# One level of Strassen in the first channel product of a fused attention and mixer kernel, with its weights streamed through a ring

## The chip, the cores and the metric

The kernel runs on one core of one Trainium2 chip. The metric is the device time of one execution in microseconds (us). The kernel before has a median of 504.48 us over 3 runs (504.46 to 504.53). Five engines work in a core: TensorE (PE, matrix products into the banks of PSUM), VectorE (DVE), ScalarE (ACT), GpSimd (POOL) and SyncE (SP, which here issues the DMAs). Each engine takes its own instructions in their written order and waits on counting semaphores.

## The reference, cut to what matters

```
attn_out = local-and-global attention(q, k, v)                # 2 batches, 8 heads, 768 tokens, 64 wide
x  = attn_out as (2, 768, 512)
h  = relu(x^T @ w_tok1) @ w_tok2                              # 768 -> 256 -> 768, over tokens
u  = x + h^T
x2 = u + relu(u @ w_ch1) @ w_ch2                              # 512 -> 1536 -> 512, over channels
theta = x2 @ w_theta
y  = w_tok_r @ (x2*cos(theta)) + w_tok_i @ (x2*sin(theta))    # over tokens
u2 = x2 + y
out = u2 + relu(u2 @ w_ch)
```

The change is in the two channel products of the third step, `u @ w_ch1` (the first) and `relu(...) @ w_ch2` (the second).

## The kernel before, in words

Every product of two fp32 matrices in these stages is made of three matmuls of fp32r operands (`three`, line 285): each operand is split into a high part (rounded by a copy) and a low part (the operand minus the high part), and high*high, high*low and low*high are added up in PSUM. Splitting is work of the other engines: POOL splits the weights (a copy at line 650, a subtraction at 651), ACT makes the high part of an activation and DVE the low part.

Work runs in this order, batch 0 then batch 1 inside each stage where not said otherwise. **Attention** (both batches, `head_scores`, `transpose_probs`, `weigh_values`). **Tokens**: `hidden_tokens` (6 tiles of 128 tokens times 2 halves j) and `mixed_tokens` (8 tiles (c, k_) of 128 channels by 384 tokens, two products each); after each tile DVE adds x in the bank (line 1114), ACT rounds it (799) and DVE makes its low part (1108). **Channels**: per batch 24 steps, one for each half c of the tokens (SC = 384 columns) and each tile f of the 1536 hidden channels. `hidden(i)` is 12 matmuls of 384 columns into bank 6 or 7; ACT applies relu and rounds (806), DVE makes the low part (1123), into a ring of three; `reduce_hidden(i - 1)` is 12 matmuls of 384 columns that add into banks 0 to 3. At the end of a half, `take_h2` (1041, out of PSUM, adding the high part of u) and `finish_x2` (1047, adding the low part) give x2. The tail of a batch's tiles (`tile_to_hi`, `tile_to_lo`) for the next stage is made inside this loop, and so is the work on the first angle (`angles(0)`, `find_angles(0)`, `multiply_x(0)`) in batch 1. **Angles and mixing**: for each of 12 tiles g, `angles(g + 1)` (12 matmuls of 512 columns) and then `mix(g)` (two halves of 24 matmuls, half of them 512 and half 256 columns wide). Beside it DVE runs `find_angles(g)` (six instructions, lines 1056 to 1066), waits for two sines of ACT (771, 772), multiplies by x (1076, two instructions), ACT rounds both products (784), DVE makes their low parts (1081) and then the low part of the tile after the next (`tile_to_lo`, 1032). `mix(0)` waits until all of `take_h2` is done. **Last channels**: `last_channels`, with POOL and DVE sharing the low parts.

The weights lie in SBUF in ten slots `wsplit` of 2 x 1536 columns; they come through two staging buffers `wraw`. SP loads chunk i when chunk i - 2 has been split (`load_weight`, 487). All of w_ch1 (4 slots) and w_ch2 (4 slots) is split once, in batch 0, and stays for batch 1. The six chunks of w_tok_r and w_tok_i are rounded by ACT (`round_tokri`, 767) in slots that come free during the last half of batch 1, with POOL's subtraction (651) behind each; the two chunks of w_ch are split by POOL in the mixing stage.

Two of the lines that the text refers to by what they read:

```
dve.tensor_tensor(tile_at(g)[:, 1]..., rows_at(act_raw[:, b], s), tile_at(g)[:, 0]..., ALU.subtract)        # 1032: both operands in SBUF
dve.tensor_tensor(lo_[:, u_cols(i)], U_BANK[i][:, 0:SC], hi[:, u_cols(i)].bitcast(F32), ALU.subtract)       # 1108: one in PSUM, one in SBUF
```

## Time and profile before

| | |
|---|---|
| median of 3 runs | 504.48 us |
| the profiled execution, its own time | 504.67 us |
| its span | 502.9 us |
| TensorE busy | 496.2 us, 99% of the span, 2977 matmuls |
| VectorE busy | 271.5 us, 54% |
| ScalarE busy | 175.5 us, 35% |
| GpSimd busy | 141.5 us, 28% |
| granted TensorE clock | 1.00 of full speed |

The span is the time from the first to the last recorded instruction; about 1.8 us of the execution lie around it. Busy times are summed per engine. The mean duration of a matmul is longer than its share of the engine's time, because matmuls are pipelined: the pace is read from the starts of groups in the timeline.

### The profile page before, as it was taken

Reading aid. Unit: us, or ns where it says so; the run is one execution under the profiler, and the core shown is the slowest. Engines: PE = TensorE matmul, PEld = TensorE weight load, DVE = VectorE, ACT = ScalarE, POOL = GpSimd, SP = SyncE. Lnnn points to the kernel's source line nnn. Section 1 sums busy time; section 2 is a strip of 40 time slices with the busy share of each in tenths; the row PEclk is TensorE's granted clock in tenths of the full one; section 3 lists DMA queues with packets and bytes.
Section 4 is the critical chain, followed back from the end, with each engine's and each line's share of the span. In section 5 each row is a group of like instructions: output and inputs, shape, how many; then the busy total and the mean of one; then the engine's idle time right before and its main releaser. Section 6 shows DMA issues by size and latency. Waiting matters only on the chain.

```text
span 502.9 us, 8110 instructions
## 1 busy us (share of the span) xinstructions
PE 496.2 (99%) x2977; PEld 467.9 (93%) x2977; DVE 271.5 (54%) x715; ACT 175.5 (35%) x375; POOL 141.5 (28%) x131
## 2 busy tenths in 40 slices
PE   7999999999999999999999999999999999999997
PEld 5999999899999999989999999998888899888897
DVE  6998998672212421075212424247787665764452
ACT  6999898541111111123111143422323320321130
POOL 3575566499900000005000041730320220000040
PEclk9999999999999999999999999999999999999999
DMA  6887774634431100002120212320001221000002
GB/s 236 321 297 246 236 216 133 204 127 134 159 98 27 45 2 0 1 0 81 45 60 4 61 30 99 125 84 1 1 2 48 61 82 64 1 0 1 1 33 94
DMA packets 24777, 43.50 MB, mean 86 GB/s; under 512 B 3104, under 2 KB 17440, under 8 KB 24736
## 3 DMA queue, kind: packets, MB, share of 16 engines
q1 hardware_dynamic: 24736, 42.96, 26.8%
q8 instruction: 24, 0.39, 0.3%
q14 instruction: 17, 0.14, 0.1%
HBM read 33.52 MB, written 3.15 MB: 73 GB/s over the span
## 4 chain that ended last, share of the span: by engine, by line
PE 97%; DVE 1%; DMA 1%; issue 0%; ACT 0%
PE bank L288 74%; PE bank L1456 7%; PE bank L1236 5%; PE bank L1266 4%; PE bank L1269 4%; PE bank L1250 2%; PE bank L1248 2%; DMA counts<-both_counts 1%; PE bank L1276 0%; DVE wsplit L875 0%; DVE wsplit L946 0%; DVE act_raw L1209 0%; ACT probsT L673 0%; ACT wsplit L680 0%; DVE scores L866 0%
## 5 line engine op out<-in xcount | busy, mean ns | idle before, releaser
L288 PE MATMUL bank<-hid,wsplit 128*128 128x384 f32 x576 | 109.2, 339 | 0.0
L288 PE MATMUL bank<-split,wsplit 128*128 128x384 f32 x576 | 109.0, 339 | 0.0
L288 PE MATMUL bank<-wsplit,zs 128*128 128x512 f32 (+1 forms) x576 | 103.3, 338 | 0.0
L288 PEld LDWEIGHTS bank<-wsplit,zs 128*128 128x128 f32 x576 | 89.8, 188 | 14.2
L288 PEld LDWEIGHTS bank<-hid,wsplit 128*128 128x128 f32 x576 | 101.9, 188 | 0.3 <-DVE hid L1123 0.2
L288 PEld LDWEIGHTS bank<-split,wsplit 128*128 128x128 f32 x576 | 102.1, 188 | 0.1
L1123 DVE SCALAR_TENSOR_TENSOR hid<-bank,hid 128x384 fp32r<-128x384 f32 x48 | 26.8, 558 | 135.7 <-ACT hid L806 135.7
L651 POOL TENSOR_TENSOR wsplit<-wraw,wsplit 128x1536 fp32r<-128x1536 f32 (+1 forms) x19 | 62.8, 3308 | 76.2 <-ACT wsplit L767 75.1
L806 ACT ACTIVATE hid<-bank 128x384 fp32r<-128x384 f32 x48 | 23.5, 490 | 146.7 <-PE bank L288 146.6
L650 POOL CAST wsplit<-wraw 128x1536 fp32r<-128x1536 f32 (+1 forms) x13 | 17.4, 1338 | 125.9 <-PE bank L288 117.3
L582 POOL TENSOR_TENSOR wsplit<-qk_raw,wsplit 64x256 fp32r<-64x256 f32 x46 | 38.0, 826 | 34.0 <-DVE wsplit L883 33.6
L660 POOL TENSOR_TENSOR split<-act_raw,split 128x384 fp32r<-128x384 f32 x12 | 12.5, 1073 | 109.5 <-ACT split L840 109.5
L724 ACT ACTIVATE probs<-scores,nmax 128x232 f32<-128x232 f32 (+1 forms) x96 | 39.9, 465 | 2.4 <-DVE nmax L987 2.2
L771 ACT ACTIVATE zb<-zb 128x512 f32<-128x512 f32 x12 | 7.6, 632 | 87.4 <-DVE zb L1066 87.4
L288 PE MATMUL bank<-wsplit,tile 128*128 128x512 f32 x144 | 35.6, 395 | 0.0
L987 DVE CUSTOM_DVE_ANT_0 scores<-bank,bias 128x232 f32<-128x232 f32 (+1 forms) x96 | 32.4, 374 | 4.9 <-PE bank L1236 4.0
L1236 PE MATMUL bank<-wsplit 128*128 128x232 f32 (+1 forms) x192 | 32.7, 292 | 2.1 <-DVE wsplit L875 1.3
L1456 PE MATMUL bank<-split,wsplit 128*128 128x384 f32 x192 | 33.9, 337 | 0.0
L1266 PE MATMUL bank<-vt,probsT 128*128 128x65 f32 x192 | 33.8, 264 | 0.1
L1456 PEld LDWEIGHTS bank<-split,wsplit 128*128 128x128 f32 x192 | 33.5, 188 | 0.2
L288 PEld LDWEIGHTS bank<-wsplit,tile 128*128 128x128 f32 x144 | 26.4, 188 | 5.5
L1269 PE MATMUL bank<-vt,probsT 104*128 104x65 f32 x160 | 30.9, 275 | 0.0
(104 smaller groups left out, 599.8 us busy)
## 6 DMA issues: line engine op xcount, KB each, us to landing
wraw<-weights SPq DMA_DIRECT2D x16, 768.0 KB, 4.1
qk_raw<-qk SPq DMA_DIRECT2D x23, 528.0 KB, 4.3
vt<-v SPq DMA_DIRECT2D x10, 520.0 KB, 4.7
xT<-turned SPq DMA_DIRECT2D x64, 48.0 KB, 2.0
out<-act_raw SPq DMA_DIRECT2D x16, 192.0 KB, 1.9
wraw<-weights SPq DMA_DIRECT2D x4, 512.0 KB, 3.4
xT<-turned_early SPq DMA_DIRECT2D x16, 96.0 KB, 2.3
xT<-wraw SPq DMA_DIRECT2D x32, 48.0 KB, 1.9
```

The costliest lines, as they stand in the source:

```text
L288: mm = pe.matmul(dst, lhs(a), rhs(c), start=first and i == 0, stop=last and i == 2, skip_group_check=True)
L582: pool.tensor_tensor(q_split[D:P, n % 2, heads], q_in[D:P, n % 2, heads], q_split[D:P, n % 2, heads].bitcast(F32), ALU.subtract).then_inc( ...
L650: link(pool.tensor_copy(w_at(slot, 0, 0, width), raw))
L651: pool.tensor_tensor(w_at(slot, 1, 0, width), raw, w_at(slot, 0, 0, width).bitcast(F32), ALU.subtract).then_inc(w_ready, 1)
L724: act.activation(probs[:, n % 2, h, first:], scores[:, m % 2, e, first:], ACT.Exp, bias=nmax[:, n % 2, h:h + 1], scale=-1.0).then_inc(exp_ ...
L806: act.activation(r1s[:, i % 3, 0], bank[6 + i % 2][:, 0:SC], ACT.Relu).then_inc(r1_hi, 1)
L987: dve.tensor_tensor_reduce(out=scores[:, m % 2, e, first:], in0=S_BANK[m % 2][e][:, first:WIN], in1=bias[:, h, first:], scale=-SCALE, scal ...
L1123: dve.scalar_tensor_tensor(r1s[:, i % 3, 1], bank[6 + i % 2][:, 0:SC], 0.0, r1s[:, i % 3, 0].bitcast(F32), ALU.max, ALU.subtract).then_inc ...
L1236: mm = pe.matmul(S_BANK[m % 2][e][:, first:WIN], q_split[:, n % 2, h, :], k_split[:, i, h, key:key + WIN - first], start=i == 0, stop=i == 1)
L1266: mm = pe.matmul(dst, probsT[:, m % 2, at + P:at + 2 * P], vt[:, n % 2, 0, cols], start=m % 2 == 0 and e == 0, stop=n % T == 0, skip_group ...
L1269: mm = pe.matmul(dst, probsT[0:SEEN, m % 2, at:at + P], vt[0:SEEN, n % 2, 1, cols], start=False, stop=True, skip_group_check=True)
L1456: return pe.matmul(bank[at][:, 0:SC], w_at(CHAN_AT[k_ // 2], w, k_ % 2 * DM + d * P, P), S_(u, k_, c * SC, SC), start=first, stop=last, sk ...
```

## The change

Notation: a pair i is the two hidden tiles i and i + 6 (PAIR_F = 6 pairs). The first product of a pair over all 768 tokens is a 2 x 2 block product: the pair's two tiles by the two halves of the 512 input channels, times the two halves of the input channels by the two halves c of the tokens.

- Pair 0 of each batch is computed as before, in four products of 12 matmuls (`REGULAR`). Pairs 1 to 5 use Winograd's form of Strassen's algorithm: seven products of 6 matmuls of 384 columns instead of 48 matmuls, in banks 6 and 7.
- The four sums T1 to T4 of the blocks of u (8 tiles of 128 x 384) are made once a batch: DVE finds each (`find_sum`), ACT rounds it (`sum_to_hi`), DVE makes its low part (`sum_to_lo`). ACT copies six of the tiles of u out of PSUM for that (`u_raw`).
- The four sums of the weights are made for each pair by POOL in `split_first` (4 additions of 256 columns, copies of 768 and 1024 columns, subtractions of 768 and 1024).
- The results are put together by DVE (four additions a pair) before relu: p1 is copied out by ACT; u2, u3 and c22 are written to SBUF, the other two to PSUM. ACT's relu and DVE's low part follow, four of each a pair as before. The low part of c22 reads two operands in SBUF.
- The second product goes over all 768 tokens in blocks of six matmuls, three of 512 and three of 256 columns, into banks 0 to 5; one block of pair i - 1 stands behind each of the seven products of pair i. `take_h2` and `finish_x2` are 8 each a batch (512 and 256 columns) in place of 8 of 384.
- The weights of a pair (1024 columns of w_ch1, 1024 of w_ch2) are streamed through rings of two places, once for each batch, so they are loaded and split twice. The chunks of w_theta come between pairs 1 and 2 of batch 1.
- `angles(0)` stands behind the last of the products of batch 1, ahead of the last eight blocks. `find_angles(0)`, `sines(0)` and `multiply_x(0)` move behind it. The first two `round_tokri` are done there too, the other four one by one in the mixing stage, between `z_to_hi(g, 1)` and `tile_to_hi`.

```diff
+            def split_first(n, raw):
+                if n % PAIR_F == 0:
+                    link(pool.tensor_copy(mixes(n, 0, 0, 4), raw))
+                    return pool.tensor_tensor(mixes(n, 1, 0, 4), raw, mixes(n, 0, 0, 4).bitcast(F32), ALU.subtract)
+                a11, a12, a22, a21 = (raw[:, q * 2 * P:(q + 1) * 2 * P] for q in range(4))
+                s1, s2, s3, s4 = (mix_raw[:, q] for q in range(4))
+                link(pool.tensor_tensor(s1, a21, a22, ALU.add))
+                pool.tensor_tensor(s3, a11, a21, ALU.subtract)
+                link(pool.tensor_tensor(s2, s1, a11, ALU.subtract))
+                pool.tensor_copy(mixes(n, 0, 0, 3), raw[:, 0:3 * 2 * P])
+                link(pool.tensor_tensor(s4, a12, s2, ALU.subtract))
+                sums = mix_raw[:, :].rearrange("p q c -> p (q c)")
+                link(pool.tensor_copy(mixes(n, 0, 3, MIXES), sums))
+                pool.tensor_tensor(mixes(n, 1, 0, 3), raw[:, 0:3 * 2 * P], mixes(n, 0, 0, 3).bitcast(F32),
+                                   ALU.subtract)
+                return pool.tensor_tensor(mixes(n, 1, 3, MIXES), sums, mixes(n, 0, 3, MIXES).bitcast(F32),
+                                          ALU.subtract)
...
-                if slot < CH2:
-                    act.wait_ge(r1_ready, CHS - NF + 3 * (slot - CH1 + 1))
-                else:
-                    act.wait_ge(h2_done, CHS - NF + 3 * (slot - CH2 + 1))
+                act.wait_ge(r1_ready, B * PRODUCTS)
+                act.wait_ge(h2_done, B * BLOCKS - 2 * KD)
...
                     act.activation(split[:, 0, u_cols(i)], U_BANK[i][:, 0:SC], ACT.Copy).then_inc(uT_hi, 1)
+                    if i < 6:
+                        act.activation(u_raw[:, i], U_BANK[i][:, 0:SC], ACT.Copy).then_inc(u_copied, 1)
+                    if i == 5:
+                        sum_to_hi(0)
+                        sum_to_hi(1)
...
+            round_tokri(0)
+            round_tokri(1)
+            sines(0)
+            z_to_hi(0, 0)
...
                     z_to_hi(g, 1)
+                    if g + 2 < len(TOKRI_AT):
+                        round_tokri(g + 2)
                     if g + 2 < B * T:
                         tile_to_hi(B * T + g + 2)
...
                 for i in range(OUTB):
                     dve.wait_ge(h_ready, b * OUTB + i + 1)
                     dve.tensor_tensor(by_quads(U_BANK[i][:, 0:SC]), by_quads(U_BANK[i][:, 0:SC]), xT_at(i),
                                       ALU.add).then_inc(u_done, 1)
-                    if i:
+                    if i and i != 6:
                         lo_of_u(i - 1)
+                    if i == 5:
+                        lo_of_u(5)
+                        find_sum(0)
+                        find_sum(1)
+                    if i == 6:
+                        sum_to_lo(0)
                 lo_of_u(OUTB - 1)
+                sum_to_lo(1)
+
+                for i, (f, c) in enumerate(REGULAR):
+                    if i < 3:
+                        find_sum(2 * i + 2)
+                        find_sum(2 * i + 3)
+                    dve.wait_ge(r1_hi, b * PARTS + i + 1)
+                    dve.scalar_tensor_tensor(r1_at(b * PAIR_F, f, 1, c * SC, SC), bank[6 + i % 2][:, 0:SC], 0.0,
+                                             r1_at(b * PAIR_F, f, 0, c * SC, SC).bitcast(F32), ALU.max,
+                                             ALU.subtract).then_inc(r1_lo, 1)
+                    if i < 3:
+                        sum_to_lo(2 * i + 2)
+                        sum_to_lo(2 * i + 3)
...
+            find_angles(0)
+            take_h2(B - 1, 0)
+            take_h2(B - 1, 1)
+            multiply_x(0)
+            z_to_lo(0, 0)
+            for i in range(2, 2 * KD):
+                take_h2(B - 1, i)
             z_to_lo(0, 1)
             tile_to_lo(B * T + 2)
-            for d in range(KD):
-                finish_x2(B - 1, NC - 1, d)
+            for i in range(2 * KD):
+                finish_x2(B - 1, i)
...
+                for i, (f, c) in enumerate(REGULAR):
                     if f == 0:
                         pe.wait_ge(uT_lo, b * OUTB + (c + 1) * KD)
+                    if i >= 2:
+                        pe.wait_ge(r1_lo, b * PARTS + i - 1)
...
+                for i in range(1, PAIR_F):
+                    wait_weight(pair_in_order(b, i, 0))
+                    pe.wait_ge(r1_lo, parts - 1)
+                    product(i, 0, 6, quarter(0, 0), False)
+                    block(i - 1, *blocks[0])
+                    pe.wait_ge(p1_copied, m + 1)
+                    product(i, 1, 6, quarter(2, 0), True)
+                    block(i - 1, *blocks[1])
+                    pe.wait_ge(r1_lo, parts)
+                    pe.wait_ge(t_lo, b * SUMS + 6)
+                    product(i, 4, 7, summed(2), False)
+                    block(i - 1, *blocks[2])
...
+                if b == B - 1:
+                    angles(0)
+                for d in range(KD):
+                    block(PAIR_F - 1, 1, d)
```

## Rows read from the trace of the kernel before

**Rows 1.** The page: busy time by engine, granted clock by slice, the chain that ended last.

```profile
PE 496.2 (99%) x2977; PEld 467.9 (93%) x2977; DVE 271.5 (54%) x715; ACT 175.5 (35%) x375; POOL 141.5 (28%) x131
...
PEclk9999999999999999999999999999999999999999
...
PE 97%; DVE 1%; DMA 1%; issue 0%; ACT 0%
```

**Rows 2.** Groups of PE instructions, shapes apart: the two channel products.

```profile
L288 PE MATMUL bank<-hid,wsplit 128*128 128x384 f32 x576 | 109.2, 339 | 0.0
L288 PE MATMUL bank<-split,wsplit 128*128 128x384 f32 x576 | 109.0, 339 | 0.0
```

**Rows 3.** Timeline of PE: start us, us, then the merged instructions.

```profile
1.45 5.22 PE L1276 MATMUL bank<-wsplit 128*128 128x512 f32 x13 [1.45 <-DVE wsplit L853]
...
110.57 4.40 PE L288 MATMUL bank<-split,wsplit 128*128 128x384 f32 x24
...
142.37 2.28 PE L288 MATMUL bank<-split,wsplit 128*128 128x384 f32 x12
144.49 2.28 PE L288 MATMUL bank<-hid,wsplit 128*128 128x384 f32 x12
...
345.06 2.97 PE L288 MATMUL bank<-wsplit,tile 128*128 128x512 f32 x12
347.87 8.64 PE L288 MATMUL bank<-wsplit,zs 128*128 128x512 f32 x48
356.34 2.97 PE L288 MATMUL bank<-wsplit,tile 128*128 128x512 f32 x12
```

**Rows 4.** Timeline of DVE behind the mixing of batch 0.

```profile
106.14 0.56 DVE L1108 TENSOR_TENSOR split<-bank,split 128x384 fp32r<-128x384 f32 x1
106.61 0.56 DVE L1114 TENSOR_TENSOR bank<-bank,xT 128x384 f32<-128x384 f32 x1
...
111.72 1.21 DVE L1108 TENSOR_TENSOR split<-bank,split 128x384 fp32r<-128x384 f32 x2
```

**Rows 5.** Groups of ACT instructions, shapes apart.

```profile
L799 ACT ACTIVATE split<-bank 128x384 fp32r<-128x384 f32 x16 | 7.8, 492 | 11.7 <-DVE bank L1114 11.7
L767 ACT ACTIVATE wsplit<-wraw 128x1536 fp32r<-128x1536 f32 x6 | 8.9, 1479 | 2.9 <-DMA wraw<-weights 2.9
```

**Rows 6.** Groups of POOL instructions, shapes apart.

```profile
L651 POOL TENSOR_TENSOR wsplit<-wraw,wsplit 128x1536 fp32r<-128x1536 f32 x15 | 52.5, 3505 | 75.8 <-ACT wsplit L767 75.1
L651 POOL TENSOR_TENSOR wsplit<-wraw,wsplit 128x1024 fp32r<-128x1024 f32 x4 | 10.3, 2570 | 0.3
L650 POOL CAST wsplit<-wraw 128x1024 fp32r<-128x1024 f32 x4 | 4.2, 1042 | 117.3 <-PE bank L288 117.3
L611 POOL TENSOR_TENSOR wsplit<-wraw,wsplit 128x256 fp32r<-128x256 f32 x5 | 3.6, 727 | 0.4
```

**Rows 7.** Timelines of DVE and POOL where the two met: batch 1's channel stage.

```profile
298.67 1.31 DVE L1032 TENSOR_TENSOR tile<-act_raw,tile 128x512 fp32r<-128x512 f32 x1
...
295.92 3.52 POOL L651 TENSOR_TENSOR wsplit<-wraw,wsplit 128x1536 fp32r<-128x1536 f32 x1 [59.03 <-ACT wsplit L767]
```

**Rows 8.** Timelines of DVE and POOL where the two met: mixing stage.

```profile
353.91 2.90 DVE L1076 TENSOR_TENSOR zb<-xT,zb 128x512 f32<-128x512 f32 x1
...
353.52 2.73 POOL L651 TENSOR_TENSOR wsplit<-wraw,wsplit 128x1024 fp32r<-128x1024 f32 x1
```

**Rows 9.** Timeline of DVE, POOL idle or beside it: one step of the mixing stage, first to last.

```profile
337.05 1.96 DVE L1047 TENSOR_TENSOR act_raw<-act_raw,split 128x384 f32<-128x384 f32 x4
338.93 0.68 DVE L1056 TENSOR_SCALAR za<-bank 128x512 f32<-128x512 f32 x1
...
342.28 0.43 DVE L1066 TENSOR_SCALAR zb<-zb 128x512 f32<-128x512 f32 x1
344.02 0.69 DVE L1076 TENSOR_TENSOR zc<-xT,zc 128x512 f32<-128x512 f32 x1 [1.31 <-ACT zc L772]
...
346.62 0.69 DVE L1032 TENSOR_TENSOR tile<-act_raw,tile 128x512 fp32r<-128x512 f32 x1
```

More of the change, by code:

```diff
@@ L78, with pair_chunks, pair_in_order @@
 BORROWED = 5
-ORDER = [0, 1, 2, 6, 3, 7, 4, 8, 5, 9] + list(range(10, 20))
+def pair_chunks(first, last):
+    return [n for i in range(first, last) for n in (2 + 2 * i, 3 + 2 * i)]
+ORDER = ([TOK1, TOK2] + pair_chunks(0, PAIR_F) + pair_chunks(0, 2) + [THETA, THETA + 1]
+         + pair_chunks(2, PAIR_F) + list(range(TOKRI, CHAN + 2)))
+THETA_IN = ORDER.index(THETA)
+TOKRI_IN, CHAN_IN = ORDER.index(TOKRI), ORDER.index(CHAN)
+def pair_in_order(b, i, second):
+    return 2 + 2 * PAIR_F * b + 2 * i + second + (2 if b and i >= 2 else 0)
 BESIDE = [1, 3]
@@ L1050, in find_angles @@
             def find_angles(g):
-                theta = bank[6 if g else 4][:, :]
+                theta = bank[6][:, :]
                 dve.wait_ge(th_ready, g + 1)
@@ L1394, in _, with block @@
-                hidden(0)
-                for i in range(1, CHB):
-                    hidden(i)
-                    reduce_hidden(i - 1)
-                    if b == B - 1 and i == EARLY:
-                        angles(0)
+                def block(i, f, d):
+                    n = b * PAIR_F + i
+                    first, last = i == 0 and f == 0, i == PAIR_F - 1 and f == 0
+                    if d == 0:
+                        wait_weight(pair_in_order(b, i, 1))
+                        pe.wait_ge(r1_lo, b * PARTS + 2 * NC * i + (3 + f if i == 0 else 4 - f))
+                    if first:
+                        pe.wait_ge(t_lo, b * SUMS + 5 + d)
+                    three(pe, bank[d][:, :], lambda a: second_at(n, a, f * DM + d * P, P),
+                          lambda a: r1_at(n, f, a, 0, 512), first, last)
+                    mm = three(pe, bank[4 + d // 2][:, d % 2 * 256:(d % 2 + 1) * 256],
+                               lambda a: second_at(n, a, f * DM + d * P, P),
+                               lambda a: r1_at(n, f, a, 512, S - 512), first and d % 2 == 0, last)
+                    mm.then_inc(h2_done, 1)
@@ new lines, in product, with quarter, summed @@
+                def product(i, mix, at, rhs, more):
+                    for kk in range(2):
+                        mm = three(pe, bank[at][:, 0:SC], lambda a: mix_at(b * PAIR_F + i, a, mix, kk),
+                                   lambda a: rhs(a, kk), kk == 0 and not more, kk == 1)
+                    mm.then_inc(r1_ready, 1)
+                def quarter(k_, c):
+                    return lambda a, kk: S_(a, k_ + kk, c * SC, SC)
+                def summed(t):
+                    return lambda a, kk: sum_at(t, kk, a)
@@ L1403, in _ @@
                     hidden_tokens(b + 1, 0, 1).then_inc(tile_used, 1)
[L1404 removed]
+                for d in range(KD):
+                    block(PAIR_F - 1, 0, d)
             def mix(g):
```

424 lines of the change are left out of this document (280 added, 144 removed).

## The prediction, made blind

> **What bounds the kernel now.** I read the page's busy times and its chain first, then the groups of PE by shape, and last the timelines of the engines at the places that the change touches. TensorE is busy for 99% of the span and is 97% of the chain that ended last [rows 1]: the kernel is one unbroken stream of matmuls. So a removed matmul is worth its whole pace, and any new wait of TensorE is paid in full. Everything else is hidden at present: VectorE 54%, GpSimd 28%. The question is whether it stays hidden where the change puts its new work.
>
> **Removed: matmuls.** Each batch has 5 pairs with 7 x 6 = 42 matmuls in place of 48, so 5 x 6 x 2 = 60 of the 576 of the first product go [rows 2]. Twelve matmuls of 384 columns start 2.12 us apart (142.37 to 144.49), 0.1767 us each [rows 3]: 60 x 0.1767 = **-10.6 us**. The second product keeps its 576 matmuls, half now 512 and half 256 wide; 48 matmuls of just that mix took 8.47 us (347.87 to 356.34), 0.1765 each [rows 3]. So no change there: 0, and if the alternation costs or saves 1%, 2 us either way over the whole channel stage.
>
> **Streaming the weights.** Per pair GpSimd has four additions of 256 columns (4 x 0.73), copies of 768 and 1024 (about 0.8, between the 1024 copy's 1.04 and nothing, and 1.04), subtractions of 768 and 1024 (about 1.9, by the columns, and 2.57), then w_ch2's 1.04 + 2.57 [rows 6]: 12.9 us. TensorE's pair takes 15 groups of six at 1.06, 15.9 us. It fits, with 3 us to spare, and the loads are behind it. In the pair loop I cost it at 0; if GpSimd came to need 16 us or more, TensorE would wait the excess in each of 10 pairs.
>
> **What GpSimd does to VectorE.** This is the cost that the plan of the kernel doesn't show. A VectorE subtraction with both operands in SBUF, normally 0.69 us, took 1.31 us at 298.67: GpSimd's subtraction ran from 295.92 to 299.44, and VectorE ended 0.54 us after that [rows 7]. The one at 353.91 took 2.90 us, GpSimd being busy to 356.25 [rows 8]. So such an instruction waits until the GpSimd instruction is over. With an operand in PSUM nothing of the kind happens: those at 106 to 112 us run at 0.55 beside a busy GpSimd [rows 4]. The Trainium skill, page "SBUF — State Buffer", section "SBUF: two separate sides", puts it as an exclusive lock on a shared port pair, held for a whole instruction by whichever started first, for VectorE instructions with two SBUF inputs or in a two-port mode; by that rule the one-input fp32 steps of the angles would be held too, and none of this kernel's PSUM readers. The trace agrees.
>
> **The join in front of pair 1 (twice).** Now: tiles of u come out in VectorE steps of 0.47 us, and mixing ends at 110.57 with the four regular products (4 x 2.12) behind it [rows 3, 4]. After: ACT does two instructions a tile (2 x 0.46) for six tiles; each low part of u waits for the second, so the VectorE period grows from 0.93 to about 1.0: some 0.5 us. VectorE then has two sums more before the last two tiles and two low parts, so the 8th low part is done near 115.4 in place of 112.9, and behind it come one low part, two sums and the first relu's low part: 4 x 0.47 + 0.1 = 2.0, so 117.4. Product 3 of the four needs bank 6 back, and would start at 110.57 + 4.24 = 114.8: 2.7 us late. Behind it each product is paced by VectorE's five instructions, 5 x 0.47 = 2.33 against 2.12: 0.2 each, twice. So 3.1 us a batch with no interference. Two of these low parts (T1's) have both operands in SBUF, and GpSimd works at just this time: on pair 1's weights in batch 0, on w_theta in batch 1 (it waits for the last mixed tile). Each can be held for 0 to 2.57 us. I take 1 us in batch 0 and 2.4 us in batch 1: **+4.0 and +5.5 us**; ends 3.1 and 8 each.
>
> **The pair loop.** VectorE has 8 instructions in 15.9 us and every one has at least two groups (2.1 us) between product and deadline. The low part of c22 has two SBUF operands and can be held 2.6 us; its successors have about 3 us. One or two short waits, and at the change of batch the token tiles (two SBUF operands) meet w_ch1 of pair 1 being split: together **+1.0 us** (0 to 3).
>
> **The entrance to mixing.** Before, the first angle's work lay inside the loop, under the channel products. After, with L the end of batch 1's products: `angles(0)` ends at L + 2.8 (2.81 us, rows 3 give 345.06 to 347.87), eight blocks at L + 11.3, `angles(1)` at L + 14.1, where `mix(0)` could start [rows 3]. ACT rounds two chunks first (2 x 1.48), and GpSimd's two subtractions of 3.5 us each then run from L + 1.7 to L + 8.8 [rows 5, 6, 7], over the whole of `find_angles(0)` (3.8 us when free [rows 9]), whose steps are held. It ends near L + 11 in place of L + 6.8; then sines 1.4, products, a low part, and the six takes that are left (2.6 us), at L + 17: **+3.0 us**. With no holding: angle to L + 6.8, two takes behind blocks to L + 10, products and low part to L + 12.2, the six takes to L + 14.8, so 0.6. Then the low part of the second half is held by the next subtraction (2.4), and eight finishing additions (3.7 us) stand where four took 1.9 [rows 9], all before `find_angles(1)`. `mix(1)` waits **+3.2 us** (with none: from L + 14.8, 1.4 of low parts, 3.7, 3.8, 1.4 and 2.1 make L + 27.2, against TensorE's 14.8 + 8.5 + 2.8 = 26.1, about 1).
>
> **Steps 1 to 3 of mixing.** VectorE's step is 3.8 (angle) + 1.4 (sines) + 2.7 (products, low parts) + tile, 8.3 us in all, in TensorE's 11.28 (345.06 to 356.34) [rows 3, 9]. After, ACT puts a 1.48 us rounding ahead of `tile_to_hi`, and GpSimd's 3.5 us subtraction has started 0.6 us before the tile's low part, which reads SBUF twice: it is held 3.0 us. That is the very situation of rows 7. The step becomes about 12.7 us, and with no slack left from `mix(1)` TensorE waits 1.45 us for steps 2 and 3: **+2.9 us**.
>
> **Steps 4 and 5.** The two chunks of w_ch (1.04 + 2.57 each) were hidden in steps 2 and 3; now they follow directly on the last subtraction, 7.2 us of GpSimd over an angle whose steps take 3.8 us and mostly read SBUF twice. Between 0 and 7.2; I take **+5.0 us**, the greater part, since VectorE's step is already the longer one there.
>
> **Sum**: -10.6 + 4.0 + 5.5 + 1.0 + 3.0 + 3.2 + 2.9 + 5.0 = +14.0. The profiled execution took 504.67 us (span 502.9 and 1.8 around it), 0.2 over the median of 504.48. 504.5 + 14.0 = **518.5 us**. With the upper ends (+16.0, +3, +3.0, +3.2, +2.9, +7.2 less 10.6) it is 529, and with all lower ends of a held VectorE about 508.
>
> **Rivals.**
> (a) VectorE is hardly ever held where it counts: the instants fall between GpSimd's instructions, or VectorE gets in first. For it: the kernel before lives with a hold of 2.2 us at 353.91 [rows 8] without a wait of TensorE. Against: the rounding puts GpSimd ahead in every step. Then 2 x 3.1 for the joins + 0.6 + 0.8 to 1 = 7.6 against 10.6: -3.0 us, 501.5 us, faster. This is the other side; it decides wherever less than 3 us of holding reaches TensorE.
> (b) Also the joins are hidden, the saving stands whole: 494 us. Against: the 16 extra VectorE instructions a batch are between TensorE and its banks.
> (c) Gaps cost the clock. It is in the top tenth in all 40 slices, and TensorE idles only 6.7 us of the span in all (502.9 - 496.2) [rows 1]; after the idle start 13 matmuls of 512 columns took 5.22 us, 0.40 each, against 0.234 later [rows 3]: about 2.2 us lost by a cold restart. Four gaps of 3 us or more would give 518.5 + 8.8 = 527 us. The Trainium skill, page "TensorE: Matmul & The Clock Gate", says that an idle array falls back to half its clock; this trace has no gap in its body long enough to show it.
> (d) It doesn't do what it says: the streamed GpSimd work, held in its turn by VectorE, outgrows the pair. Ten waits of 1 to 2 us, 530 us or more.
>
> **Chances.** Forecast 0.64, (a) 0.16, (b) 0.06, (c) 0.08, (d) 0.06. The forecast's own range is 508 to 528; the range 500 to 528 takes in (a) and most of (c) as well and leaves out (b) and (d). Faster by over 0.2% (1 us, about what a measurement of this kernel can tell): (a), (b) and a little of the forecast's lower end, 0.24; within 0.2%: 0.05; slower: 0.71.
>
> **What would show it.** Matmuls of 384 columns down by 60, plus the second product's 576 turned into 288 of 512 and 288 of 256. Waits of TensorE on VectorE at the third regular product of each batch, and on the low parts of the halves in mixing. VectorE rows of the tile's low part and of the angle far over 0.69 us, each ending just behind a GpSimd subtraction. The end of the channel stage about even with before (-10.6 + 10.5), and the whole loss behind it. If these rows keep 0.69 us, the forecast is wrong; if TensorE waits inside the pairs, it is (d); if granted clock falls below 1.00, (c).

## The result and the profile after

The changed kernel takes **531.25 us** (median of four runs, 529.45 to 532.06) against 504.50 for the kernel before in the same session: ratio 1.0525, 95% interval 1.0509 to 1.0540. The prediction was 518.5 us, range 500 to 528: the sign was right, the loss was about twice the size (26.8 us where 14.0 were summed), and the result lies outside the range. The profiled execution took 532.06 us, its span is 529.9.

From the page of the changed kernel: busy times, granted clock in 40 slices, and the chain that ended last. They answer to [rows 1].

```profile
PE 498.4 (94%) x2917; PEld 452.9 (85%) x2917; DVE 354.9 (67%) x797; ACT 192.0 (36%) x413; POOL 242.5 (46%) x223
...
PEclk9999999997999999987999999998998999999999
...
PE 76%; DVE 16%; issue 4%; ACT 3%; DMA 1%; DVEq 0%; ACTq 0%
```

Sixty matmuls are gone (2977 to 2917), and TensorE is still busy for 2.2 us more than before: part of its work runs at a lower clock (the digits below 9 in the row of PEclk). VectorE, which had 1% of the chain, has 16%. Where TensorE waits, the timeline of PE says (start, us, instructions; in brackets the idle time ahead and what ended it). These are all the waits from the first channel product to the end of the first mixing stage; the kernel before has none there.

```profile
120.97 8.16 PE L324 MATMUL bank<-split,wsplit 128*128 128x384 f32 x30 [6.18 <-DVE wsplit L1302]
...
221.11 1.66 PE L324 MATMUL bank<-tile,wsplit 128*128 128x512 f32 x6 [0.84 <-DVE tile L1070]
...
225.31 1.18 PE L324 MATMUL bank<-tile,wsplit 128*128 128x512 f32 x3 [2.54 <-DVE tile L1070]
...
247.97 7.87 PE L324 MATMUL bank<-split,wsplit 128*128 128x384 f32 x30 [4.84 <-DVE wsplit L1302]
...
350.60 8.71 PE L324 MATMUL bank<-wsplit,zs 128*128 128x512 f32 x48 [2.66 <-DVE act_raw L1185]
359.63 3.04 PE L324 MATMUL bank<-wsplit,tile 128*128 128x512 f32 x12 [0.32 <-issue]
...
364.99 10.26 PE L324 MATMUL bank<-wsplit,zs 128*128 128x512 f32 x48 [2.31 <-DVE zs L1225]
...
390.05 8.71 PE L324 MATMUL bank<-wsplit,zs 128*128 128x512 f32 x48 [0.72 <-DVE zs L1225]
...
406.82 18.80 PE L324 MATMUL bank<-wsplit,zs 128*128 128x512 f32 x96 [5.25 <-DVE zs L1225]
```

The waits add up to 25.7 us: 11.0 in the two joins, 3.4 at the change of batch, 11.3 in the mixing stage. Read by stage, from the same timelines of both kernels (time after less time before, the saved matmuls counted apart): first join +9.1, change of batch +5.5, second join +7.7, the ten pairs within 0.4 of the time for 60 matmuls less, so that the channel stage ends 11.2 us later (at 344.97 for 333.79); the mixing stage of batch 0 costs another 15.6, the rest of the kernel nothing.

The joins cost more than their waits because the clock falls. Here are stretches of the changed kernel (busy us of PE, PEld, DVE, ACT, POOL with instructions, then granted clock, DMA share, GB/s): the wait of the first join and what follows, a stretch behind the change of batch, and the place behind the wait of the second join.

```profile
115.00:121.00 6.00, 0.03 (x1) 0.06 (x1) 5.90 (x9) 1.93 (x5) 3.94 (x3) 0.92 0.42 119
121.00:125.00 4.00, 4.00 (x13) 4.00 (x14) 4.00 (x9) 1.23 (x3) 0.00 (x0) 0.50 0.20 83
...
227.00:230.00 3.00, 3.00 (x10) 2.29 (x10) 0.69 (x1) 0.60 (x1) 0.00 (x0) 0.62 0.17 68
...
248.00:252.00 4.00, 4.00 (x13) 4.00 (x14) 4.00 (x9) 1.23 (x3) 0.00 (x0) 0.50 0.18 72
```

And the same for whole stages: first join, change of batch, second join, mixing of batch 0.

```profile
102.00:132.00 30.00, 23.82 (x119) 23.25 (x119) 22.15 (x38) 12.82 (x29) 20.19 (x18) 0.89 0.22 70
205.00:239.00 34.00, 30.48 (x150) 25.70 (x149) 21.64 (x34) 7.81 (x16) 16.71 (x13) 0.95 0.15 47
239.00:258.00 19.00, 14.16 (x67) 13.71 (x66) 14.58 (x27) 7.76 (x19) 9.78 (x8) 0.82 0.17 56
345.00:428.00 83.00, 71.74 (x361) 59.84 (x360) 68.50 (x96) 25.85 (x40) 24.05 (x11) 0.96 0.18 53
```

Behind a wait of 5 to 6 us the granted clock is 0.50, the level of 1.2 GHz: 13 matmuls in 4.00 us, where 0.1767 us each [rows 3] would give 22.6. That is 1.7 us lost in each join in these 4 us alone. In all the clock costs about 10.6 us (an estimate: in stretches of 1 us, one less the granted clock, times TensorE's busy time): 3.0 in the first join, 1.7 at the change of batch, 2.6 in the second join, 3.3 in mixing. Busy time says the same: the 2917 matmuls take 498.4 us here and 486.9 in experiment H, whose page shows a clock of 1.00 throughout, 11.5 us less. Waits and clock (25.7 + 10.6) less the saved matmuls (11.3) make 25.0 of the 26.8.

VectorE does not pace the products behind the wait in the first join. It idles there for ScalarE, which waits for TensorE:

```profile
125.71 0.56 DVE L1302 SCALAR_TENSOR_TENSOR wsplit<-bank,wsplit 128x384 fp32r<-128x384 f32 x1 [0.69 <-ACT wsplit L919]
...
125.19 0.49 ACT L919 ACTIVATE wsplit<-bank 128x384 fp32r<-128x384 f32 x1 [1.97 <-PE bank L324]
```

What holds VectorE in the first join, in its timeline and in that of GpSimd:

```profile
113.07 2.62 DVE L1278 TENSOR_TENSOR wsplit<-t_raw,wsplit 128x384 fp32r<-128x384 f32 x1
...
117.20 2.23 DVE L1278 TENSOR_TENSOR wsplit<-t_raw,wsplit 128x384 fp32r<-128x384 f32 x1
```

```profile
112.90 2.38 POOL L716 TENSOR_TENSOR wsplit<-mix_raw,wsplit 128x1024 fp32r<-128x1024 f32 x1
115.23 1.37 POOL L720 CAST wsplit<-wraw 128x1024 fp32r<-128x1024 f32 x1
116.67 2.35 POOL L721 TENSOR_TENSOR wsplit<-wraw,wsplit 128x1024 fp32r<-128x1024 f32 x1
```

Both low parts of T1 have their two inputs in SBUF. Free, such a low part takes 0.55 us (at 113.08 in A below); here each ends 0.4 us behind a GpSimd subtraction (115.69 behind 115.28; 119.43 behind 119.02). It is the meeting of [rows 7, 8], and GpSimd was at 1024-column subtractions both times.

### The profile page after: what moved, and what is told of

Read it like the earlier page. It is cut to its first block, busy times and chain, and to the rows that moved or that the text cites. A ratio compares the mean times of both kernels' runs of the same rounds, so it can differ in the third digit from the quotient of the medians.

```text
span 529.9 us, 8302 instructions
## 1 busy us (share of the span) xinstructions
PE 498.4 (94%) x2917; PEld 452.9 (85%) x2917; DVE 354.9 (67%) x797; ACT 192.0 (36%) x413; POOL 242.5 (46%) x223
## 4 chain that ended last, share of the span: by engine, by line
PE 76%; DVE 16%; issue 4%; ACT 3%; DMA 1%; DVEq 0%; ACTq 0%
PE bank L324 54%; PE bank L1715 6%; PE bank L1452 4%; PE bank L1482 4%; PE bank L1485 3%; PE bank L1466 2%; PE bank L1464 2%; DVE wsplit L1278 1%; DVE act_raw L1191 1%; DVE zb L1205 1%; DVE bank L1284 1%; DVE split L1251 1%; DVE tile L1070 1%; ACT wsplit L870 1%; DVE zs L1225 1%
## 5 line engine op out<-in xcount | busy, mean ns | idle before, releaser
L324 PE MATMUL bank<-wsplit 128*128 128x512 f32 (+2 forms) x816 | 148.9, 338 | 0.0
L324 PEld LDWEIGHTS bank<-wsplit 128*128 128x128 f32 x816 | 134.5, 188 | 13.6 <-DVE wsplit L1327 0.2
L324 PE MATMUL bank<-wsplit,zs 128*128 128x512 f32 (+1 forms) x576 | 106.8, 346 | 10.9 <-DVE zs L1225 8.3
L324 PEld LDWEIGHTS bank<-wsplit,zs 128*128 128x128 f32 x576 | 92.0, 193 | 26.9 <-issue 12.6
L324 PE MATMUL bank<-split,wsplit 128*128 128x384 f32 x276 | 59.0, 362 | 11.1 <-DVE wsplit L1302 11.0
L324 PEld LDWEIGHTS bank<-split,wsplit 128*128 128x128 f32 x276 | 52.1, 206 | 12.1 <-issue 12.0
L757 POOL TENSOR_TENSOR wsplit<-wraw,wsplit 128x1536 fp32r<-128x1536 f32 (+1 forms) x11 | 34.5, 3138 | 52.0 <-ACT wsplit L870 51.6
L1327 DVE SCALAR_TENSOR_TENSOR wsplit<-bank,wsplit 128x384 fp32r<-128x384 f32 x30 | 16.7, 557 | 35.5 <-ACT wsplit L937 24.3
L1715 PE MATMUL bank<-split,wsplit 128*128 128x384 f32 x192 | 34.2, 339 | 0.0
L1715 PEld LDWEIGHTS bank<-split,wsplit 128*128 128x128 f32 x192 | 33.8, 188 | 0.2
L720 POOL CAST wsplit<-wraw 128x1024 fp32r<-128x1024 f32 x12 | 13.3, 1107 | 40.1 <-PE bank L324 40.1
L721 POOL TENSOR_TENSOR wsplit<-wraw,wsplit 128x1024 fp32r<-128x1024 f32 x12 | 29.6, 2467 | 1.0
```

The costliest lines, as they stand in the source:

```text
L324: mm = pe.matmul(dst, lhs(a), rhs(c), start=first and i == 0, stop=last and i == 2, skip_group_check=True)
L720: link(pool.tensor_copy(second_at(n, 0, 0, 2 * DM), raw))
L721: return pool.tensor_tensor(second_at(n, 1, 0, 2 * DM), raw, second_at(n, 0, 0, 2 * DM).bitcast(F32), ALU.subtract)
L757: pool.tensor_tensor(w_at(slot, 1, 0, width), raw, w_at(slot, 0, 0, width).bitcast(F32), ALU.subtract).then_inc(w_ready, 1)
L1327: dve.scalar_tensor_tensor(r1_at(n, f, 1, off, SC), src, 0.0, r1_at(n, f, 0, off, SC).bitcast(F32), ALU.max, ALU.subtract).then_inc(r1_lo, 1)
L1715: return pe.matmul(bank[at][:, 0:SC], w_at(CHAN_AT[k_ // 2], w, k_ % 2 * DM + d * P, P), S_(u, k_, c * SC, SC), start=first, stop=last, sk ...
```

## The experiments

Nine kernels, each timed against the kernel before on the same chip (504.38 to 504.48 us there).

| kernel | us (lowest to highest) | ratio to before, 95% |
|---|---|---|
| the change | 531.25 (529.45 to 532.06) | 1.0509 to 1.0540 |
| A GpSimd out of the joins | 519.76 (519.49 to 519.97) | 1.0270 to 1.0327 |
| B mixing stage mended | 522.82 (519.46 to 524.28) | 1.0290 to 1.0393 |
| C no late low parts | 516.08 (513.21 to 517.44) | 1.0166 to 1.0260 |
| D Strassen undone | 520.56 (519.73 to 521.02) | 1.0280 to 1.0342 |
| E as A, joins turned | 521.32 (520.65 to 523.45) | 1.0304 to 1.0341 |
| F E with mixing mended | 507.93 (507.61 to 510.28) | 1.0048 to 1.0106 |
| G D with mixing mended | 505.46 (505.13 to 505.51) | 1.0004 to 1.0024 |
| H F, joins turned again | 499.93 (499.61 to 502.29) | 0.9908 to 0.9943 |
| I H with GpSimd let in | 508.29 (507.30 to 509.97) | 1.0067 to 1.0101 |

**A. GpSimd kept out of the joins and the change of batch.** It waits, and works later in the pairs. For that, w_theta had to go behind the last pair in the order of the chunks.

```diff
-ORDER = (... + pair_chunks(0, 2) + [THETA, THETA + 1] + pair_chunks(2, PAIR_F) + ...)
+ORDER = (... + pair_chunks(0, PAIR_F) + [THETA, THETA + 1] + ...)
+                if n == 1:
+                    pool.wait_ge(t_lo, 1)
...
+                        if n == PAIR_F + 1:
+                            pool.wait_ge(x2_done, 2 * KD)
...
+                        if n % PAIR_F == 1:
+                            pool.wait_ge(t_lo, n // PAIR_F * SUMS + 2)
```

> Edit: GpSimd's splits are kept out of the two joins and of the change of batch, by waits of GpSimd on VectorE's progress (the last subtraction of pair 1's w_ch1 waits for the first low part of T1, pair 1's w_ch2 for the second, in batch 1 pair 1's w_ch1 for the end of finish_x2), and w_theta moves behind the last pair. Nothing of the computation changes. Theory (holds of VectorE by GpSimd in the joins, and the clock that they cost): no VectorE subtraction over 0.7 us in the joins, waits of TensorE there 6.2 and 4.8 down to about 2.7 each, the waits of 0.8 and 2.5 us on token tiles gone, less time at the lower clock: 531.3 - 3.7 - 2.1 - 3.4 - 3 (clock) = about 519 us. Rival (the joins are long because VectorE has too many instructions, whoever runs beside it): waits of 6 and 5 us stay, over 529 us.

Measured 519.76, 11.5 us under the change. The waits at the change of batch are gone, those of the joins shrink but stay:

```profile
117.57 5.92 PE L324 MATMUL bank<-split,wsplit 128*128 128x384 f32 x30 [2.76 <-DVE wsplit L1308]
...
235.86 6.78 PE L324 MATMUL bank<-split,wsplit 128*128 128x384 f32 x30 [4.01 <-DVE wsplit L1308]
```

So GpSimd's work at these places, that of w_theta among it, is 11.5 us of the loss here, the clock that falls with it included (TensorE's busy time is 493.1 us for 498.4). A join without it still has a wait. The order of VectorE's own work is the suspect; E and H test it.

**B. The mixing stage mended, the rest as in the change.** Each streamed subtraction of GpSimd waits until VectorE's step is through its two-input work, ScalarE takes a token tile's high part ahead of a rounding, and both halves of the turned columns come at step 5.

```diff
                         pool.wait_ge(w_hi, chunk - TOKRI + 1)
+                        if chunk == TOKRI:
+                            pool.wait_ge(ang_done, 2)
+                        elif chunk == TOKRI + 1:
+                            pool.wait_ge(z_lo, 1)
+                        else:
+                            pool.wait_ge(tile_lo, B * T + chunk - TOKRI + 2)
...
-                    if g + 2 < len(TOKRI_AT):
-                        round_tokri(g + 2)
                     if g + 2 < B * T:
                         tile_to_hi(B * T + g + 2)
+                    if 1 <= g < len(TOKRI_AT) - 1:
+                        round_tokri(g + 1)
```

> Edit: only the mixing stage. ACT makes the next tile's high part before it rounds a chunk, chunks 2 to 5 are rounded one step later, and GpSimd's subtractions wait for VectorE's progress (the first for the end of the first angle, the second for the first low part, the others for the low part of a tile), so that they run where VectorE has slack. The two waiting transposes go together behind step 5. Nothing of the computation changes. Theory (15.6 us of the loss is GpSimd holding VectorE in this stage): waits of TensorE in the stage 11.3 down to 1 to 3 us, tile low parts at 0.69 us, 531.3 - 11 = about 520 us. Rival (the stage is long because the first angle's work and the roundings were moved into it): no more than 4 us gained, over 527 us.

Measured 522.82, with runs 4.8 us apart. The waits of 11.3 us in mixing fell to 3.9 (0.86, 1.64, 1.44), and one of 2.64 us came up behind them, because both halves of the turned columns now waited at step 5 for the last two weights (VectorE idled 3.70 and 1.57 us there for GpSimd). So 6.6 us of waits are left where 1 to 3 were expected: this version of the mend had a queue of its own.

**C. The late low parts left out.** The low parts of the token weights of mixing and of the w_ch chunks are set to zero by a memset, so the products with them are still made, with zeros.

```diff
+                    if TOKRI <= chunk:
+                        pool.memset(w_at(slot, 1, 0, width).bitcast(F32), 0.0).then_inc(w_ready, 1)
+                    else:
...
                     pool.tensor_tensor(w_at(slot, 1, 0, width), raw,
```

> Edit: GpSimd's subtraction of 1536 or 1024 columns for the chunks of w_tok_r, w_tok_i and w_ch is replaced by a memset of the same columns to zero, which reads no SBUF. This leaves out the low parts of these weights. All orders and waits stay. Theory (holds): the VectorE instructions of 3.6, 3.1, 2.5 and 2.0 us in the entrance and the mixing stage return to 0.69 and 0.43, TensorE's waits there fall from 11.3 to 1 to 2 us, about 518 us. Rival (order of work, not the lock): VectorE's rows may shorten but the waits keep over two thirds, over 527 us.

Measured 516.08. The waits of mixing fell from 11.3 us to 1.0 (0.43 and 0.57), those of the joins stayed at 6.32 and 5.01. Nothing else in the mixing stage changed, its order least of all: its loss is GpSimd's subtraction beside VectorE. The memset is also shorter (1.38 us for 3.47), but VectorE's steps run free beside it too. Here is the tile's low part of step 1, the one that took 3.61 us in the change, inside a memset:

```profile
360.80 0.69 DVE L1172 TENSOR_TENSOR tile<-act_raw,tile 128x512 fp32r<-128x512 f32 x1 [1.20 <-ACT tile L864]
...
360.36 1.38 POOL L758 MEMSET wsplit<- 128x1536 f32 x1 [13.18 <-ACT wsplit L873]
```

**D. Strassen alone undone.** Four products of twelve matmuls a pair again, no sums; the streaming, the 512 and 256 columns of the second product and all moved steps stay.

```diff
-        PRODUCTS = 2 * NC + 7 * (PAIR_F - 1)
+        PRODUCTS = 2 * NC * PAIR_F
...
-                        sum_to_hi(2 * i + 2)
-                        sum_to_hi(2 * i + 3)
...
-                        find_sum(2 * i + 2)
-                        find_sum(2 * i + 3)
...
+                    for j, (f, c) in enumerate(REGULAR):
```

> Edit: Strassen alone is undone. All six pairs of a batch use four products of 12 matmuls; the sums of u, the copies for them, the sums of weights and the joining additions are gone. All tokens at once, blocks of 512 and 256 columns, the streamed weights, the moved angle and the moved roundings stay. 60 matmuls more than the changed kernel. Theory: joins cost nothing (-16.7 us), matmuls cost 10.6, the change of batch costs 2 in place of 5.5, the mixing stage keeps its 15.6: 531.3 - 16.7 + 10.6 - 3.5 = about 522 us. So Strassen by itself loses 6 to 9 us here, and the streaming and moving lose the rest. Rival (the loss lies in Strassen alone): back near 505 us. Rival (the loss lies in streaming and moving alone): Strassen is a gain of 10.6 and this kernel takes 540 us.

Measured 520.56: no wait in the joins, 1.43 at the change of batch, 11.2 in mixing. So streaming and moved steps cost 16 us by themselves, and Strassen adds 10.7 to them where it should take 10.6 off.

**E. As A (without its first wait, which the third one covers), with the joins turned.** The regular products' low parts come ahead of the sums on VectorE, and ScalarE begins the sums behind the first regular part.

```diff
-                        sum_to_hi(2 * i + 2)
-                        sum_to_hi(2 * i + 3)
+                    sum_to_hi(2 * i)
+                    sum_to_hi(2 * i + 1)
...
+                    if i in (1, 2):
+                        find_sum(2 * i - 2)
+                        find_sum(2 * i - 1)
...
+                    if i == 2:
+                        for n in range(4, SUMS):
+                            find_sum(n)
+                        for n in range(2, 5):
+                            sum_to_lo(n)
```

> GpSimd kept out of both joins and the change of batch as in the first experiment of this study (which read 519.8), and in addition the order of the join turned on ScalarE and VectorE: the two low parts of the regular products come before the sums they were queued behind, the low parts of the third to eighth sum behind them. Theory (in a join without GpSimd what TensorE waits for is the place of a regular low part behind 4 to 6 VectorE instructions of 0.47 us for the sums): the join waits of 2.76 and 4.01 fall to about 1 each, nothing is left of the low clock there, time 513 to 515. Rival (VectorE's total of 18.5 us in a join against 17.0 of TensorE is the bound, whatever the order): the waits only move, 2 to 3 us in each join, time 517 to 519.

Measured 521.32: the theory missed, and so did the rival. It is no faster than A (1.6 us slower by the medians, though the intervals against the kernel before overlap). The waits of both joins come to 6.4 us for A's 6.8. The long wait became two, and the clock fell behind them for longer:

```profile
119.83 1.28 PE L324 MATMUL bank<-split,wsplit 128*128 128x384 f32 x6 [0.77 <-DVE wsplit L1299]
123.38 2.26 PE L324 MATMUL bank<-wsplit 128*128 128x512 f32 x6 [2.27 <-DVE wsplit L1279]
```

```profile
122.00:126.00 4.00, 2.62 (x8) 2.37 (x9) 3.09 (x7) 0.75 (x2) 3.79 (x6) 0.59 0.38 125
126.00:130.00 4.00, 4.00 (x15) 3.71 (x15) 0.56 (x1) 0.49 (x1) 3.97 (x2) 0.56 0.00 0
130.00:134.00 4.00, 4.00 (x25) 3.72 (x24) 2.35 (x4) 0.00 (x0) 0.00 (x0) 1.00 0.46 131
```

The profiled execution, 523.45 us, is the slowest of the four. VectorE was not full in this join: it idled 0.97 and 0.94 us ahead of the second and third regular low part, for ScalarE, which took them behind two sums that it was waiting for. So the order was still wrong, on the other engine.

**F and G. The mixing stage mended on E and on D.** As in B, and the last additions of the second residual spread over steps 1 to 4; one half of the columns is turned at step 5, the other behind the last angles. G also takes from A the order of the chunks and the gate at the change of batch.

```diff
-            for i in range(2 * KD):
-                finish_x2(B - 1, i)
...
                         find_angles(g)
+                        if g <= KD:
+                            finish_x2(B - 1, 2 * g - 2)
+                            finish_x2(B - 1, 2 * g - 1)
...
-                    if b == 0 and s >= T - 2:
-                        dve.wait_ge(w_ready, len(ORDER))
...
+                    if b == 0 and s == T - 1:
+                        turn_half(0)
...
                     find_angles((b + 1) * T)
+                    turn_half(1)
```

> The kernel with the turned order in the joins, GpSimd kept out of joins and change of batch, and the mixing stage mended too: each low part of a token weight waits until VectorE has the angles or low parts of its step, one rounding a step is taken behind the token tile on ScalarE, the last additions of the second residual are spread over steps 1 to 4, the columns are turned at step 5 and behind the last angles. Theory (all of the loss is the VectorE held or queued, none is in the Strassen products or the streaming as such): 494 for the products without waits, plus 2 for the joins, 2 to 4 for the change of batch, 1 to 3 for the mixing stage: 500 to 504, at or under the kernel before. Rival (what the change adds in work on VectorE and GpSimd turns up as a wait somewhere else): 506 to 512.

> Strassen undone, streaming and moved steps kept (which alone read 520.6), and the mixing stage mended as in the kernel above. Theory (the moved angle and roundings and the streamed low parts, not the streaming through the ring, cost the 16 us): waits of 11.4 us in the mixing stage fall to 1 to 3, time 506 to 509. Rival (the transfers and the low parts through the ring cost several us by themselves, in the channel loop): 512 or more.

Measured 507.93 and 505.46. G settles the streaming: its time is just under the 506 to 509 expected, and with the mixing stage in order, the ring and all the moved steps cost 1.0 us over the kernel before, the clock on its page is 1.00 throughout, and its only waits behind the first channel product are 0.87 and 1.56 us. The theory for F (500 to 504) missed by 4 us, and the time lies where its rival put it (506 to 512). But mixing has the same two waits as G: what is left is 6.4 us of waits in the joins, as in E, and the clock behind them.

**H. The joins turned once more.** ScalarE takes the third regular part ahead of sums 4 to 7; VectorE takes all that the first block needs ahead of the fourth regular low part.

```diff
-                    sum_to_hi(2 * i)
-                    sum_to_hi(2 * i + 1)
+                    for n in ((), (0, 1, 2, 3), (4, 5), (6, 7))[i]:
+                        sum_to_hi(n)
...
+                    for n in ((), (0, 1, 2, 3), (4, 5), ())[i]:
+                        find_sum(n)
+                    if i == 2:
+                        sum_to_lo(0)
+                    if i == 3:
+                        sum_to_lo(1)
+                        find_sum(6)
+                        find_sum(7)
+                        for n in range(2, 5):
+                            sum_to_lo(n)
```

> The mended kernel that read 507.9, with the order of the joins turned once more: ScalarE takes the third regular part ahead of the sums it waited behind, VectorE takes what the first block of the second product needs (eight sums and five low parts) ahead of the fourth regular low part. In the mended kernel TensorE waited 0.76 and 2.27 us in the first join, 1.10 and 2.25 in the second, and ran both at the lower clock for some us behind it. Theory (the rest of what Strassen costs is this order and the clock that falls with it): from the start of the third regular low part's chain VectorE has 16 instructions of 0.47 us, 7.5 us, to the first block, against 6.7 us of TensorE: waits of 0.5 to 1.5 us a join, no low clock, time 500 to 503, faster than the kernel before. Rival (the total of VectorE's work in a join is the bound, and the clock falls at any gap there): 505 to 508.

Measured **499.93 us: 0.75% faster than the kernel before** (0.57 to 0.92) and 31 us under the change. The page's clock and the waits of TensorE behind the first channel product, all of them:

```profile
PEclk9999999999999999999999999999999999999999
```

```profile
120.81 1.29 PE L324 MATMUL bank<-wsplit 128*128 128x512 f32 x6 [0.88 <-DVE wsplit L1286]
...
236.00 1.29 PE L324 MATMUL bank<-wsplit 128*128 128x512 f32 x6 [1.34 <-DVE wsplit L1286]
...
329.16 8.73 PE L324 MATMUL bank<-wsplit,zs 128*128 128x512 f32 x48 [0.85 <-issue]
...
384.54 8.71 PE L324 MATMUL bank<-wsplit,zs 128*128 128x512 f32 x48 [1.53 <-DVE zs L1231]
```

Against F, 8.0 us came from an order alone: the same instructions (but for the semaphore waits that keep the order safe), 4.2 us less waiting, and TensorE busy for 486.9 us in place of 490.5, since the clock did not fall. That holds for four of the six executions. The other two took 501.95 and 502.29 us at a mean clock of 0.993, so the clock does fall in some executions of this kernel, and why was not tried. Against G, the same kernel without Strassen, 5.5 us of the ideal saving are left.

**I. H with GpSimd let into the joins and the change of batch.**

```diff
-                        if n == PAIR_F + 1:
-                            pool.wait_ge(x2_done, 2 * KD)
...
-                        if n % PAIR_F == 1:
-                            pool.wait_ge(t_lo, n // PAIR_F * SUMS + 2)
```

> The same kernel, but GpSimd is let into the joins and the change of batch again: it splits streamed weights there as in the change. Theory (GpSimd's casts and subtractions hold VectorE 1.5 to 2.4 us at a time, and in the join VectorE has no slack): waits grow by 2 to 5 us a join and by 2 to 5 at the change of batch, with the clock 8 to 14 us in all, time 510 to 516. Rival (with the right order the holds fall into VectorE's slack): within 2 us of its sister.

Measured 508.29: 8.4 us over H, at the low end of the 8 to 14 expected, and 1.7 under the time that stood beside it. In the joins the rival is nearer: they wait 2.55 and 1.35 us where H waits 0.88 and 1.34. At the change of batch the theory holds, 3.6 us of waits, and a clock of 0.89 from 214 to 222 us and of 0.90 from 222 to 230:

```profile
214.94 1.67 PE L324 MATMUL bank<-tile,wsplit 128*128 128x512 f32 x6 [0.84 <-DVE tile L1072]
...
219.14 0.96 PE L324 MATMUL bank<-tile,wsplit 128*128 128x512 f32 x3 [2.53 <-DVE tile L1072]
220.34 1.65 PE L324 MATMUL bank<-third,wsplit 128*128 128x512 f32 x3 [0.24 <-DVE third L1072]
```

The token tiles' low parts there took 2.29 and 2.83 us in place of 0.69, beside GpSimd at the weights of pair 1; this is the second:

```profile
216.25 2.83 DVE L1072 TENSOR_TENSOR tile<-act_raw,tile 128x512 fp32r<-128x512 f32 x1
...
215.86 2.67 POOL L721 TENSOR_TENSOR wsplit<-wraw,wsplit 128x1024 fp32r<-128x1024 f32 x1
```

## Why the prediction was wrong

Two steps failed. The sum had nothing for TensorE's clock behind its own waits, and the clock cost 10.6 us; the result lies 12.8 us over the 518.5. And two meetings of VectorE and GpSimd were priced too low: the low parts of T1 in the first join, and the token tiles at the change of batch. The mechanism, VectorE held by GpSimd where TensorE has no slack, was right. The sum of 14.0, term by term, by the same stages as above:

**The matmuls, -10.6: right.** A pair took 16.96 us before (eight groups at 2.12) and 15.80 to 15.83 after (but for one of 16.00), 1.13 less, -11.3 over ten. The blocks of 512 and 256 columns are as fast as said.

**The pair loop at 0 for streaming: right.** The low part of c22, with both inputs in SBUF, was held as foreseen; the group's mean is 1725 ns over ten, three times the 557 of its sisters with an input in PSUM, and TensorE never waited:

```profile
L1327 DVE SCALAR_TENSOR_TENSOR wsplit<-joined,wsplit 128x384 fp32r<-128x384 f32 x10 | 17.2, 1725 | 5.9 <-ACT wsplit L939 5.9
```

Rival (d) is out.

**The joins, +4.0 and +5.5: failed, for the most part by the clock.** They took +9.1 and +7.7. The place was right (the third regular product, behind 24 matmuls) and so was the mechanism. I had this product late by 3.7 and 5.1 us; it was late by 6.35 and 5.0. So batch 1 came out, and batch 0 didn't: I priced one hold there, at 1.0 us, though my own text says "Each can be held for 0 to 2.57 us". Both were, by 2.07 and 1.68 us. Behind the third product I had 0.4 us for VectorE's pace, and it took 2.7 us in each join, all of it about what the granted clock explains (3.0 and 2.6). The clock had no term in my sum.

**The change of batch, within +1.0: failed.** It took +5.5: 3.4 of waits, 1.7 of clock. Both token tiles met the weights of pair 1 and were held 1.6 and 2.1 us. I had named the meeting, and costed it together with the pair loop at 1.0. There is no slack for it: TensorE waited for both tiles. The waits are gone in A and H, and 3.6 us of them are back in I, where GpSimd is let in.

**The mixing stage, +14.1: +15.6, right in cause, and in size partly by luck.** The entrance waited 2.66 (said 3.0), the second product 0.32 + 2.31 (3.2), steps 2 and 3 0.72 (2.9), the end 5.25 (5.0): 11.3 of waits for 14.1. The clock, which I had at nothing, brought another 3.3 and made up for waits that I had priced too high, above all those of steps 2 and 3. The cause was right, since C removes just that subtraction and the waits are gone. The tile's low part was held in steps 1 to 3 as in [rows 8] (3.61, 3.66 and 3.64 us); step 1:

```profile
366.64 3.61 DVE L1169 TENSOR_TENSOR tile<-act_raw,tile 128x512 fp32r<-128x512 f32 x1 [1.20 <-ACT tile L861]
```

```profile
366.24 3.47 POOL L757 TENSOR_TENSOR wsplit<-wraw,wsplit 128x1536 fp32r<-128x1536 f32 x1 [13.40 <-ACT wsplit L870]
```

**Rivals.** (a) and (b) are out: VectorE was held at nearly every meeting, and it reached TensorE.

**Rival (c), chance 0.08, came true beside the forecast, not in place of it.** It should not have been a rival at all, but a term of the sum: my own forecast held waits of 3 us and more. Its price of 8.8 us was near the 10.6 measured, but partly by luck: the 2.2 us a gap came from the slow start of the kernel before, where the profile grants a clock of 1.00 (1.45 to 6.70 us), so that row does not show that the clock was the cause. What the page "TensorE: Matmul & The Clock Gate" of the Trainium skill says in its section "What's actually happening" of an idle array (half its clock) is now borne out by the stretches at 0.50; the trace of before could not show it.

In sum: of the 12.8 us between 518.5 and 531.3, the joins and the change of batch are 11.8 (their 22.3 less the 10.5 of my terms), the mixing stage 1.5, the matmuls -0.7. The clock's 10.6 lies in the first two, 7.3 and 3.3. I had also said that the end of the channel stage would be about even with before; it came 11.2 us later. The range left out 528 and more, though the upper ends of my own terms gave 529 without the clock; with 10.6 us for it the range would have reached 540. (The lower ends of a held VectorE, 3.1 twice and 0 at the end, add up to 509, not 508.)

**Where the expected gain went.** It is there, 11.3 us. Going back from H: 6.4 us of loss is the order in the joins (A less H, less the mixing stage), 13.4 the mixing stage (E less F), 11.5 GpSimd in the joins and at the change of batch (the change less A), each with the clock that fell with it. They add up to the 31.3 between H and the change by the way they are taken, so the sum is no check on them. The parts are measured with the others present or absent as the runs had them, and the clock makes them depend on each other, as I against A shows (8.4 and 11.5; A moves w_theta out of the second join too, where I and H both have it behind the last pair). H is still 6.7 us over the 493.2 that the matmuls alone would give (504.5 - 11.3); its four waits are 4.6 of that, 2.2 in the joins and 2.4 in mixing. They were not taken further.

## What to carry to other kernels

When an engine is at 99% and work is added to its helpers, list for each added instruction which buffers its inputs lie in, and which GpSimd instruction runs at that time: a VectorE instruction with two inputs in SBUF is worth 0.6 us or 3.6 us by that alone. A stage where the bottleneck consumes each result at once (a join, a change of batch) has no slack, and there the order on every helper in the ring counts as much as its total: the same instructions read 507.9 and 499.9 us. Price a wait of TensorE with the clock behind it (in the changed kernel 10.6 us of clock came with 25.7 of waits), and move streamed work into the stretches that are even, as a gate on GpSimd did here.

## What the hardware showed that was not expected

**The clock does not go by the length of one wait.** In A, a wait of 2.76 us left it at 1.00, and one of 4.01 us brought 0.56 in the next stretch (rows of A below). In E, waits of 0.77 and 2.27 us, whose ends are 3.6 us apart, came with 0.59 and 0.56 over 8 us; on the pages of H and G waits of 0.85 to 1.56 us left it alone. Nor does it go by the kernel alone: H took 499.6 to 500.0 us in four executions and 2 us more in two, at 0.993. What tells the cases apart was not tried.

```profile
113.00:118.00 5.00, 2.24 (x14) 1.95 (x12) 4.90 (x11) 2.91 (x7) 4.22 (x2) 1.00 0.00 0
118.00:122.00 4.00, 4.00 (x23) 3.61 (x22) 4.00 (x10) 2.27 (x5) 3.63 (x3) 1.00 0.47 131
...
235.00:238.00 3.00, 2.14 (x7) 2.17 (x8) 3.00 (x8) 2.02 (x5) 2.90 (x2) 0.56 0.00 0
```

**One-input steps are held too.** The trace of before didn't show it. In the changed kernel, the step that bounds the angle in step 4 (zb from zb, one fp32 input in SBUF) took 2.47 us at 400.81 for 0.43 when free [rows 9], and ended 0.28 us behind a GpSimd subtraction. The page "SBUF — State Buffer" of the Trainium skill (section "Who interferes with whom") counts such one-input operations, `tensor_scalar` among them, with those that can contend with GpSimd. This row agrees:

```profile
400.81 2.47 DVE L1210 TENSOR_SCALAR zb<-zb 128x512 f32<-128x512 f32 x1
...
400.31 2.69 POOL L757 TENSOR_TENSOR wsplit<-wraw,wsplit 128x1024 fp32r<-128x1024 f32 x1
```

**GpSimd is held in turn.** The cast of 1024 columns took 1.37 us at 115.23 for 1.04 [rows 6]: the VectorE low part of 113.07 ended at 115.69, 0.46 us after the cast had started. So VectorE in its turn draws out the GpSimd work that will hold it next.

**A memset of GpSimd beside the same VectorE steps held nothing that TensorE noticed** (C: 1.0 us of waits for 11.3, and 0.69 us for the tile's low part inside a memset). The same section of that page of the Trainium skill says that a VectorE instruction with two SBUF inputs contends with a GpSimd instruction that reads SBUF, not with one that only writes it. A memset reads none, and the rows of C agree.
